# Windowed and pooled attention, then two MLPs, on one core: a weight product begun two steps later

## The reference

```
# 1. attention on q, k, v of (4, 8, 576, 64): 32 heads, S = 576, D = 64
q_d, k_d, v_d = means over groups of 4 tokens            # 144 tokens
out_d     = softmax(q_d k_d^T / 8) v_d, each row repeated 4 times
out_local = softmax(q k^T / 8, only |i - j| < 4) v
x = out_d + out_local                                     # as (2304, 512)
# 2. x = ((x w1) * (x w2)) w3 w_out    w1, w2: 512x1024; w3: 1024x1024; w_out: 1024x512
# 3. h = x w_in; out = (h * sigmoid(h)) w_out2             w_in: 512x2048; w_out2: 2048x512
```

## Time and profile before

| | us |
|---|---|
| median of the runs | 842.61 |
| the profiled execution | 841.73 |
| its span | 839.9 |
| PE busy | 816.2 (97%) |
| DVE busy | 609.2 (73%) |
| ACT busy | 336.5 (40%) |
| POOL busy | 284.1 (34%) |

### The profile page before, as it was taken

How to read it: one execution, slowest core, us unless ns; L and a number is a source line. 1 busy time by engine, 2 the same in 40 slices (tenths; PEclk the granted TensorE clock), 3 DMA queues, 4 the chain that set the end, 5 groups by cost and what they waited for, 6 DMA issues and landing times.

```text
span 839.9 us, 14773 instructions
## 1 busy us (share of the span) xinstructions
PE 816.2 (97%) x5584; PEld 733.6 (87%) x5584; DVE 609.2 (73%) x976; ACT 336.5 (40%) x605; POOL 284.1 (34%) x348
## 2 busy tenths in 40 slices
PE   5899999999999999999999999999999999999998
PEld 4778888788999999999999998898898898988987
DVE  3667779887768676677768876777866778866654
ACT  3645565653225422433226333235333245333231
POOL 5876668843322432233221421320411311411100
PEclk9899999999999999999999999999999999999999
DMA  7856676211110111101112311311511311512202
GB/s 184 214 146 163 153 195 169 61 51 51 51 52 26 51 51 51 51 26 51 50 52 76 101 51 51 101 51 50 176 51 55 96 51 50 176 51 62 64 1 75
DMA packets 128731, 68.98 MB, mean 82 GB/s; under 512 B 63392, under 2 KB 117152, under 8 KB 128672
## 3 DMA queue, kind: packets, MB, share of 16 engines
q1 hardware_dynamic: 128672, 68.18, 28.6%
HBM read 63.44 MB, written 4.72 MB: 81 GB/s over the span
## 4 chain that ended last, share of the span: by engine, by line
PE 90%; DVE 5%; issue 2%; POOL 1%; ACT 0%; DMA 0%; SPq 0%; DVEq 0%; POOLq 0%
PE ps L1054 41%; PE ps L1112 24%; PE ps L1083 12%; PE ps L1213 4%; PE ps L1127 2%; PE ps L1192 2%; PE ps L1176 1%; PE ps L1137 1%; PE ps L1148 1%; PE ps L1167 1%; PE ps L1221 1%; PE ps L1159 1%; DVE wa L750 1%; DVE tr L744 1%; DVE tot L847 0%
## 5 line engine op out<-in xcount | busy, mean ns | idle before, releaser
L1054 PE MATMUL ps<-xb,wa 128*128 128x384 f32 x2016 | 405.4, 338 | 2.4 <-DVE a L882 1.4
L1054 PEld LDWEIGHTS ps<-xb,wa 128*128 128x128 f32 x2016 | 355.0, 188 | 24.6 <-DVE mu L882 2.6
L433 POOL TENSOR_TENSOR rw<-rw 128x256 f32<-128x256 f32 x48 | 42.3, 880 | 443.1 <-DMA rw<-in_moe_w_in 208.6
L882 DVE TENSOR_TENSOR mu<-ps,mu 128x384 f32<-128x384 f32 x132 | 73.3, 555 | 121.0 <-PE ps L1054 120.7
L1083 PE MATMUL ps<-g,r 128*128 128x512 f32 (+1 forms) x576 | 125.0, 338 | 1.8 <-issue 1.8
L644 ACT ACTIVATE a<-a 128x384 f32<-128x384 f32 x72 | 37.9, 526 | 188.6 <-DVE a L882 188.6
L1112 PE MATMUL ps<-w2h_even,g 128*128 128x512 f32 x432 | 113.2, 394 | 0.0
L1112 PE MATMUL ps<-w2h_odd,g 128*128 128x512 f32 x432 | 112.5, 393 | 0.0
L750 DVE TENSOR_TENSOR wa<-rw,wa 128x1024 fp32r<-128x1024 f32 x96 | 108.5, 1131 | 2.6 <-ACT wa L507 2.3
L1083 PEld LDWEIGHTS ps<-g,r 128*128 128x128 f32 x576 | 97.7, 188 | 10.4 <-issue 2.4
L1112 PEld LDWEIGHTS ps<-w2h_odd,g 128*128 128x128 f32 x432 | 79.9, 188 | 11.9
(11 more groups left out here) (86 smaller groups left out, 881.7 us busy)
## 6 DMA issues: line engine op xcount, KB each, us to landing
rw<-in_moe_w SPq DMA_DIRECT2D x48, 256.0 KB, 3.2
rw<-in_moe_w_in SPq DMA_DIRECT2D x48, 256.0 KB, 3.1
w2r<-in_moe_w_out SPq DMA_DIRECT2D x48, 256.0 KB, 2.9
qn<-in_q SPq DMA_DIRECT2D x32, 144.0 KB, 3.0
kn<-in_k SPq DMA_DIRECT2D x32, 144.0 KB, 3.2
vw<-in_v SPq DMA_DIRECT2D x32, 144.0 KB, 2.9
out<-osb SPq DMA_DIRECT2D x18, 256.0 KB, 2.4
wn<-in_moe_w SPq DMA_DIRECT2D x16, 256.0 KB, 3.0
```

What stands on the lines that cost most here:

```text
L433: nc.gpsimd.tensor_tensor(blocks[:, 4, :], blocks[:, 0, :], blocks[:, 1, :], ALU.add).then_inc(s1_ready, 1)
L882: nc.vector.tensor_tensor(o, half_bank(k, i), term, ALU.add).then_inc(sum_ready, 1)
L1054: e = nc.tensor.matmul(ps[:, (k + i) % 2, 0:TH], wa[:, k % 2, l, A_SLOT[i], a * P:(a + 1) * P], xb[:, i, r, a, :], start=(i in (0, 1, 4) a ...
```

## The change: what it does

- **Two steps later.** Piece (0, 0) is flipped in step 3 and multiplied in step 4, and every piece after it two steps later than before. Steps 1 and 2 have no flip, steps 2 and 3 no piece. The last step has four pieces, (6, 0), (6, 1), (7, 0) and (7, 1), with the two flips of m = 7 between them, where it had two pieces and no flip. Step 4 (`late_fold`) does its four parts after the probabilities' products. In the steps with h = 0 parts 0 and 1 come behind the turn of k and not ahead of it.
- **w_out split** in steps 3 and 4; of each four blocks VectorE makes two low parts and GpSimd two. It is loaded by two DMAs of four blocks.
- **First loads over two queues.** Of q and k of the pairs 0 and 1 ScalarE's queue issues the second head.
- **SP's order**: q, k and v of the pairs 2 to 4 come ahead of w3 and w_out.
- **First keys in banks of their own**: k of pair 0 is turned into pP, without a wait for `qt_ready`.
- **q is turned early** in steps 0 to 3: ahead of the wait for `exp_d`.
- **Filler turns** (`warm`): two 128x128 transposes of the identity in step 0 and six in step 1, into bank pW. (The call `warm(8)` under `if turn and not early` is never reached, since step -1 counts as early.)
- GpSimd clears `vg` ahead of the masks, so that the loads that wait for it start sooner.

The core of the diff:

```diff
             step(0, -1, True, False, False, None, None)
             step(0, 0, True, True, False, None, None)
-            step(0, 1, True, True, True, None, (0, 0))
-            step(0, 2, True, True, True, (0, 0), (0, 1))
-            with eng.Fori(1, AHEAD // 2) as i:
-                step(i, 1, True, True, True, (i - 1, 1), (i, 0))
-                step(i, 2, True, True, True, (i, 0), (i, 1))
+            step(0, 1, True, True, True, None, None)
+            step(0, 2, True, True, True, None, None)
+            step(1, 1, True, True, True, None, (0, 0))
+            step(1, 2, True, True, True, (0, 0), (0, 1))
+            with eng.Fori(2, AHEAD // 2) as i:
+                step(i, 1, True, True, True, (i - 2, 1), (i - 1, 0))
+                step(i, 2, True, True, True, (i - 1, 0), (i - 1, 1))
...
-            step(0, PAIRS - 1, False, True, True, (MT - 2, 1), (MT - 1, 0))
-            step(0, PAIRS, False, False, True, (MT - 1, 0), None)
+            step(0, PAIRS - 1, False, True, True, (MT - 3, 1), (MT - 2, 0))
+            step(0, PAIRS, False, False, True, (MT - 2, 0), None)
...
+            nc.gpsimd.memset(vg[:, :, :, :], 0.0).then_inc(blank, 1)
...
+            for s in range(2):
+                for there, here, there_in in ((qn, q_heads, q_in), (kn, k_heads, k_in)):
+                    act.dma_start(there[:, s, :, D:2 * D], here[2 * s + 1:2 * s + 2, :].rearrange("o (p a d) -> (o p) a d", p=PT, d=D)
+                                  ).then_inc(there_in[s], 16)
...
                 if last:
+                    w3_high((MT - 1, 0), pT + 1)
+                    take_w3o(MT - 2, pW)
+                    w3_high((MT - 1, 1), pT)
                     act.wait_ge(scored, 2 * PAIRS)
...
+                def w_out_low(half):
+
+                    for n in (4 * half, 4 * half + 1):
+                        dve.wait_ge(r3_hi, n + 1)
+                        nc.vector.tensor_tensor(r3[:, n, 1, :], raw3[:, n, BANK:], r3[:, n, 0, :].bitcast(F32),
+                                                ALU.subtract).then_inc(r3_lo_dve, 1)
...
                     for a in range(4):
                         multiply(a)
+                    turn_w3((MT - 1, 0), pT + 1)
+                    for a in range(4):
+                        multiply(a, (MT - 2, 1))
+                    turn_w3((MT - 1, 1), pT)
                     turn_local()
                     turn_down()
-                    multiply(0, (MT - 1, 1))
-                    multiply(1, (MT - 1, 1))
+                    for a in range(3):
+                        multiply(a, (MT - 1, 0))
                     weighted_local_waits()
-                    multiply(2, (MT - 1, 1))
-                    multiply(3, (MT - 1, 1))
+                    multiply(3, (MT - 1, 0))
                     weighted_local()
                     weighted_down()
+                    for a in range(4):
+                        multiply(a, (MT - 1, 1))
                     return
+                first, early = not score, isinstance(s, int) and s < FOLD
+                if early:
+                    if s == 0:
+                        pe.wait_ge(qt_ready, 1)
+                    else:
+                        pe.wait_ge(kt_ready, s + 1)
+                    pe.wait_ge(q_in[n], 32 * h1 + 32)
+                    turn_in(qn, q_turned)
+                    warm((2, 6, 0, 0)[s])
...
+            def warm(n):
+                for _ in range(n):
+                    nc.tensor.transpose(ps[:, pW, 0:P], ident[:, :], ident[:, :])
```

More of the change, by code:

```diff
@@ L168, in attention_then_mlps @@
         wn_in = [sem(f"wn_in{h}") for h in range(2)]
-        r3_in = [sem(f"r3_in{n}") for n in range(MT)]
+        r3_in = [sem(f"r3_in{n}") for n in range(2)]
         rw_in = [sem(f"rw_in{n}") for n in range(2)]
@@ L273, in load_q @@
                     sp.wait_ge(q_turned, s - 1)
-                for h in range(2):
+                for h in range(1 if first else 2):
                     sp.dma_start(qn[:, u, :, h * D:(h + 1) * D],
@@ L601, in step @@
                     exps_down()
-                if isinstance(s, int) and s in (1, 2):
-                    for m in range(MT // 2 * (s - 1), MT // 2 * s):
-                        act.wait_ge(r3_in[m], 16)
+                if isinstance(s, int) and s in (FOLD - 1, FOLD):
+                    half = s - FOLD + 1
+                    act.wait_ge(r3_in[half], 16)
+                    for m in range(MT // 2 * half, MT // 2 * (half + 1)):
                         copy_act(r3[:, m, 0, :], raw3[:, m, BANK:]).then_inc(r3_hi, 1)
[L606 to L611, removed]
+                if mul and mul[1] == 1:
+                    take_w3o(mul[0], pW)
                 if score and not turn:
-                    w3_high((MT - 1, 1), pT)
+                    w3_high((MT - 2, 1), pT)
                 if last:
@@ L1201, in multiply @@
                     m, h = mul
-                    last = not turn and not score
+                    last = isinstance(m, int) and m == MT - 1
                     if part == 0:
@@ L1247, in step @@
                     scores_local()
-                if turn:
+                if turn and not early:
+                    if first:
+                        warm(8)
                     pe.wait_ge(q_in[n], 32 * h1 + 32)
@@ L1252, in step @@
                     scores_local()
+                late_fold = isinstance(s, int) and s == FOLD
                 if weigh:
                     turn_local()
[L1255 to L1257 removed]
+                    if mul and mul[1] == 1:
+                        if turn:
+                            multiply(0)
+                        multiply(1)
                 if turn:
                     pe.wait_ge(k_in[n], 32 * h1 + 32)
[L1260 to L1261 removed]
+                    if first:
+                        turn_in(kn, k_turned, pP)
+                    else:
+                        pe.wait_ge(qt_ready, s + 2)
+                        turn_in(kn, k_turned)
+                if weigh and mul and mul[1] == 0 and not late_fold:
+                    multiply(0)
+                    multiply(1)
                 if weigh:
```

99 lines of the change are left out of this document (63 added, 36 removed).

## The result

The changed kernel took 844.8 us (median of 18 runs, 843.16 to 848.85) against 841.45 us (18 runs, 839.82 to 846.11): ratio 1.0042, 95% interval 1.0028 to 1.0055. It is slower by 3.4 us where 7.2 us faster was forecast. The profiled execution is the longest of the 18: 848.85 us, span 847.1.

What follows compares the result with a forecast made beforehand. PE's own work was taken to bound the kernel behind step 5, chains of dependences ahead of it. Terms: -13.2 at step 5, +6.85 in step 16, -0.8 at the MLP's head, sum -7.15, so 835.4 us; range 831.5 to 840.5.

Steps and rivals of the forecast that it cites:

- Start to step 1: Kernel start to the scores of pair 1: these come at 14.9 us against 18.3, a gain of 3.4.
- Steps 2 to 4: First steps: step 2 ends at 29.2 us, step 3 at 36.3, step 4 at 46.5; 2.5 added gives 49.0.
- SP needs 7.5 us of issue for a step's loads, so the queue doesn't yet fall behind: Steps 2 and 3: SP's load queue keeps up, so no wait for loads was added.
- Rival (d): Loads don't start sooner, or q4 to q6 come late with SP's queue at its limit: 1 to 2 us; no own chance.
- I get the probabilities ready 9.9 us into the step and PE there at 9.9: Step 16: a tie between probabilities and PE, costing 0 to +1.5 us, taken as +0.2.
- 6.85 - 0.8 = 6.05: Behind step 15: step 16 costs 6.85 us more, the head of the MLP 0.8 less.
- a hole above 1.5 us in the last step: Step 16: one of the signs that would show the prediction wrong.
- The head of the MLP: Behind step 16: product 6 is held less than before, -0.8 us (0 to -1.4).
- Steps 5 to 15: Middle stretch, bound by PE: 103.05 us unchanged, -0.7 to +0.7 taken as 0.
- the 2.5 us that the sum added for such things: Ahead of step 5: 2 us for a drop of the clock and 0.5 for handovers.
- Rival (b): Delay follows w_out's work: free steps take 9.0 us, steps 4 and 5 12.5 each; 845.6 us, chance 0.09.

Runs made afterwards that it cites:

- e6: Kernel e4 with all low parts of w_out on GpSimd, as in the kernel before the change: 841.35 us, ratio 0.9990 to the kernel before.
- e1: The changed kernel unaltered, run and profiled again: 845.6 us, ratio 1.0040 to the kernel before.
- e2: The changed kernel with the loads of q and k of pair 6 moved ahead in SP's queue: 841.9 us, ratio 0.9996 to the kernel before.
- e5: Kernel e4 with the second heads of q and k of pairs 4 to 15 issued by ScalarE's queue: 837.9 us, ratio 0.9953 to the kernel before.
- e4: The changed kernel with both edits, those of e2 and e3: 841.3 us, ratio 1.0001 to the kernel before.
- e3: The changed kernel with the sum of m = 6 in the second bank of pS instead of pW: 842.85 us, ratio 1.0010 to the kernel before.
- g1: Kernel f1 with q and k of pair 4 loaded ahead of w_out's second half: 833.2 us, ratio 0.9901 to the kernel before.
- g2: Kernel e8 with q and k of pair 4 loaded ahead of w_out's second half: 836.3 us, ratio 0.9932 to the kernel before.
- e8: The changed kernel without the two-step delay, SP's loads nearly in the order of before: 836.2 us, ratio 0.9934 to the kernel before.
- f1: Kernel e8 with the second heads of q and k of pairs 4 to 15 issued by ScalarE's queue: 837.0 us, ratio 0.9947 to the kernel before.

## Why the prediction was wrong

**Start to step 1: the path right, 1.3 us short.** The first turn came at 4.60 (forecast 4.2, before 4.48), the scores of pair 1 at 16.23 (14.9, before 18.25), so 2.0 us were gained and not 3.4. Where I took 0.3 for the second queue there was none: ScalarE issued at 0.74, ahead of its table, but with four loads issued at once one takes 3.9 to 5.5 us (medians to landing) where it took 3.1 to 3.3. And k of pair 0, which now waits for no copy, waits 0.67 for its own load, a term that the sum had at nothing.

**Steps 2 to 4: near, the wait missed.** Step 2 ends at 30.9, step 3 at about 39, step 4 at 50.8, where my sum with its additions had 49.0. Of that 1.15 is the wait for GpSimd's normalising: it takes 2.11 us beside VectorE's two low parts (1.26 us from 41.72), and 1.14 before and in e6, where VectorE makes none. I had read the rule of the Trainium skill (SBUF — State Buffer, Who interferes with whom) for the low parts alone and found no change to the sum; the row shows what it does to the operation ahead of them:

```profile
41.88 2.11 POOL L487 TENSOR_TENSOR prob_d<-prob_d,invd 72x576 f32<-72x576 f32 x1 [1.08 <-DVE invd L900]
```

**The step that failed first: "SP needs 7.5 us of issue for a step's loads, so the queue doesn't yet fall behind".** I added up issues at their undisturbed price and took only the steady step; and even so 7.5 us is more than the 6.0 and 7.1 us that the same sum gave steps 2 and 3. In the stretch that counts, SP has w3 and both halves of w_out as well, its issues are stretched (4.16 for 2.0), and q of pair 6 stands behind twenty-one of them. Rival (d) named it and gave it 1 to 2 us. It cost 4.0 at step 5 in one profile and 2.9 in e1, 2.5 more at 132 us in the first, and there the clock behind both. Taking it away shows it: e2 gains 3.7 on e1, and e5 3.4 on e4.

**The second: step 16, "I get the probabilities ready 9.9 us into the step and PE there at 9.9".** That tie held (3.27 for twelve matmuls around it). What I missed is the first instruction: `multiply` with h = 0 waits for `w3o_lo`, the sum of the m before taken out of pW. In all other steps PE has turns and scores to do in that time; before, step 16 wrote to pS. In step 16 nothing stands ahead: 1.77 us and, in the slower profile, 1.6 more at the slow clock (4.58 for 3.01). e3 shows 2.0 in the profile and 2.7 in the median. The prediction's own sign, a hole above 1.5 us in the last step, came true. With the hole mended the price behind step 15 is 6.2 us (e5), where the sum had 6.85 - 0.8 = 6.05: the rest of that term was right.

**The head of the MLP: right.** From the end of step 16 to product 6: 8.1 us, 8.7 before, -0.5 (forecast -0.8). **Steps 5 to 15** kept their price without the waits: 94.4 us from step 5 to step 15's mark in e1, 94.3 before.

**How far each step was off, by e1.** Its span is 842.3, and the forecast's was 834.6 - 1.8 = 832.8: 9.5 us. Of these, 6.3 stand at step 5 (55.33 for 49.0). 2.9 are the wait for q, and 3.4 lie in the steps ahead of it: 1.2 at the scores of pair 1 (16.14), the rest behind, where PE was at 1.2 GHz from 28 to 33 us and waited 1.14 for the normalising; the 2.5 us that the sum added for such things were too little. 2.2 come from step 15 to product 6, 0.9 behind it and 0.1 between. So the queue alone doesn't make up the miss.

**The slower rival's number is luck.** Rival (b) had 845.6, and the kernel took 844.8. But (b) wanted steps 2 and 3 at 9.0 us and steps 4 and 5 at 12.5; the first turns of steps 2, 3 and 4 are 7.4 and 8.7 apart, step 5 takes 9.1 in e1, and the two holes are in none of its terms.

**The balance of the delay, which the sum never made alone.** I worked out one start for step 5 for the whole change and set all of it against 6.65 us behind. Had I priced the delay by itself, the question would have been how much of the 6.65 the first steps give back. Measured with the loads out of the way, 2.6 (e5 against g1): steps 2 and 3 without pieces are bound by the exponentials, the normalising and then step 4's own handovers. That these bind there is read from the waits of 0.4 to 1.15 us in the rows above; no run took them apart. So even with both faults mended the delay loses 4 to 5 us. As it was made it cost 9, and turned the 5.5 us that the rest of the change brings into a loss of 3.4.

Open: what part of the rest's gain is order, queues or banks, whether the fillers do anything, and the stretch behind product 6, 657.9 us here and 657.2 before, which lies between 657.0 and 658.4 in all the profiles.

## What to carry to other kernels

Price every part of a change by itself, above all work moved out of an idle place to a full one: it costs its whole length where it goes, and gives back only what the place that it leaves was bound by. When steps get shorter, add up the issuing queue's time for the very stretch that gets short, with all one-time loads in it, and look at what stands ahead of the load that is needed next. For work moved to the head of a step, read the waits of its first instruction again: what hid them was the work that used to stand ahead.

## What the runs showed of the hardware

- A DMA issue has no fixed price: four issues for v took 2.0 us and, where the 16 DMA engines were full (share 1.05), 4.16 on the same queue. The first landing didn't gain from a second queue (4.4 to 5.0 us in all kernels with it, 4.48 before), but in the steady steps moving two of a step's thirteen issues to ScalarE's queue removed the waits for q with the same bytes (e5, from step 7 on). The Trainium skill (DMA: Bandwidth & Descriptors, Issuing engines are not separate DMA queues) calls the issue time that a second queue saves usually small next to the DMA itself; here it is worth 3.4 us, because the queue that issues was the bound (about 25.6 us of issue in 28 in e4). Without the delay it was worth 3.1 with one order of loads (g2 to g1) and nothing with another (e8 to f1).
- A hole of 1.77 us was followed by 1.2 GHz in one execution (twelve matmuls 4.58 us) and one of 1.75 us at the same place was not in another (3.01).
- A GpSimd multiply of two tensors (72x576, f32) took 2.11 us beside two subtractions of VectorE that read two tensors each, and 1.14 us without them (e6).
